# Inverting the softmax sums of three head pairs as 128x9, gathered and spread by transfers

## The reference, cut to what matters

```python
B, H, S, D = 4, 8, 576, 64
scores = q @ k^T / 8 + min(bias(s), 0), causal
attn = exp(scores - max(scores, -1))
attn = attn / (sum(attn, -1) + 1e-9)           # the division that the change is about
x = attn @ v                                    # [B, S, 512]
h = relu(x @ w_in); conv_out = conv over 3 rows of h
x = (h * sigmoid(conv_out)) @ w_out             # 1024 hidden columns
u = x + (x^T @ U @ V)^T
out = u + relu(u @ w_ch1) @ w_ch2               # 2048 hidden columns
```

## Time and profile before

| | us |
|---|---|
| median of 3 runs (998.87 to 1003.27) | 1002.07 |
| the profiled execution | 999.37 |
| its span, first to last instruction | 997.6 |

### The profile page before, as it was taken

How to read it: one execution, slowest core, us unless ns; L and a number is a source line. 1 busy time by engine, 2 the same in 40 slices (tenths; PEclk the granted TensorE clock), 3 DMA queues, 4 the chain that set the end, 5 groups by cost and what they waited for, 6 DMA issues and landing times.

```text
span 997.6 us, 16111 instructions
## 1 busy us (share of the span) xinstructions
PE 929.6 (93%) x6455; PEld 868.0 (87%) x6455; DVE 531.9 (53%) x913; ACT 350.8 (35%) x670; POOL 5.9 (1%) x20
## 2 busy tenths in 40 slices
PE   2898898979999899999999999999999989999998
PEld 1676788968999799987999999987999989889998
DVE  5459896346775583346554784146655670342222
ACT  1365564444333443433332453332332331211111
POOL 1000000000000000000000000000000000000000
PEclk9799997989999799999999999999999999999999
DMA  4677455735564646533645546433555434344441
GB/s 93 137 213 189 110 165 171 214 101 157 179 205 153 180 127 211 191 120 129 186 163 170 169 130 207 154 112 113 177 169 169 170 127 162 127 136 173 167 162 58
DMA packets 68257, 155.68 MB, mean 156 GB/s; under 512 B 30356, under 2 KB 44692, under 8 KB 55896
## 3 DMA queue, kind: packets, MB, share of 16 engines
q1 hardware_dynamic: 68184, 154.66, 49.9%
HBM read 114.57 MB, written 30.03 MB: 145 GB/s over the span
## 4 chain that ended last, share of the span: by engine, by line
PE 75%; DVE 13%; issue 3%; ACT 3%; DMA 2%; SPq 2%; ACTq 0%; DVEq 0%
PE psum L1019 20%; PE psum L1021 18%; PE psum L1020 18%; PE psum L996 8%; PE psum L942 3%; PE psum L975 2%; DVE sums L746 2%; PE psum L973 2%; DVE neg_max L733 2%; DVE work L784 2%; DVE work L787 2%; PE psum L956 1%; DVE work L782 1%; DMA klc<-cum_scratch 1%; DVE ring L844 1%
## 5 line engine op out<-in xcount | busy, mean ns | idle before, releaser
L1019 PE MATMUL psum<-r_hl,ring 128*128 128x288 f32 x512 | 157.7, 308 | 3.8 <-DVE work L816 1.9
L1019 PE MATMUL psum<-uu_hl,ring 128*128 128x288 f32 x512 | 155.8, 304 | 3.1 <-DVE ybuf L806 1.7
L1021 PE MATMUL psum<-r_hl,ring 128*128 128x288 f32 x512 | 152.2, 297 | 0.0
L1020 PE MATMUL psum<-r_hl,ring 128*128 128x288 f32 x512 | 152.2, 297 | 0.0
L1021 PE MATMUL psum<-uu_hl,ring 128*128 128x288 f32 x512 | 151.3, 296 | 0.0
L1020 PE MATMUL psum<-uu_hl,ring 128*128 128x288 f32 x512 | 151.2, 295 | 0.0
L733 DVE TENSOR_REDUCE neg_max<-psum 128x1 f32<-128x512 f32 (+4 forms) x165 | 83.1, 538 | 117.6 <-PE psum L947 110.9
L825 DVE SCALAR_TENSOR_TENSOR r_hl<-psum,r_hl 128x288 fp32r<-128x288 f32 x128 | 58.2, 456 | 154.5 <-ACT r_hl L646 154.3
L996 PE MATMUL psum<-probs,va 128*128 128x320 f32 (+4 forms) x448 | 126.0, 392 | 0.4 <-ACT probs L572 0.4
L646 ACT ACTIVATE r_hl<-psum 128x288 fp32r<-128x288 f32 x128 | 52.4, 411 | 203.8 <-PE psum L1021 203.8
L1019 PEld LDWEIGHTS psum<-r_hl,ring 128*128 128x128 f32 x512 | 97.6, 191 | 7.3 <-DVE work L816 3.1
(11 more groups left out here) (96 smaller groups left out, 1717.4 us busy)
## 6 DMA issues: line engine op xcount, KB each, us to landing
ring<-w_scratch SPq DMA_DIRECT2D x72, 1024.0 KB, 4.9
w_scratch<-ring SPq DMA_DIRECT2D x24, 1024.0 KB, 5.3
kq_raw<-in_kq_t SPq DMA_DIRECT2D x70, 288.0 KB, 4.4
stage<-in_w_ch SPq DMA_DIRECT2D x16, 512.0 KB, 6.7
khc<-khh SPq DMA_DIRECT2D x34, 144.0 KB, 2.3
qm<-qhl SPq DMA_DIRECT2D x34, 144.0 KB, 2.5
out_t<-u_acc SPq DMA_DIRECT2D x16, 288.0 KB, 2.1
va<-in_v SPq DMA_DIRECT2D x34, 128.0 KB, 3.8
```

The costliest lines, as they stand in the source:

```text
L1019: pe.matmul(o, hi, m_hi, start=start, stop=False)
L1020: pe.matmul(o, hi, m_lo, start=False, stop=False)
L1021: return pe.matmul(o, lo, m_hi, start=False, stop=stop)
```

## The change

For pairs 0, 1 and 2 each head's sums now leave PSUM as one row of 576 (one partition instead of 64). SP cuts the rows of the two heads into 64 pieces of 9 and puts them on 128 partitions (`gather_sums`); DVE inverts that 128x9 tile (`invert_few`); SP stores it to DRAM (`store_few`), waits until it is there, and reads each head's row back to all 64 partitions of its half (`spread_few`, two transfers); DVE multiplies the pair's 128x576 at once (`normalise_few`). Pair 3 keeps its two halves with the old code. `sums` has two buffers instead of four, and the split of pair 2 moves from step (7, 1) to (7, 2).

The places: `gather_sums` at step 0 of heads 1 to 6 on SP; `invert_few` in DVE's `then` at step 2 of heads 2, 4 and 6, ahead of `query_low`; `store_few` at step 3 of these heads, behind `load`; `spread_few` at step 4, ahead of `load_v`; `normalise_few` in `then` at step 1 of heads 3, 5 and 7.

```diff
+        few = [sb(f"few{i}", [P, SP9], F32) for i in range(2)]     # SP9 = S // D = 9
+        spread_out = sb("spread_out", [P, S], F32)
-        sums = sb("sums", [P, NPAIR, S], F32)
+        sums = sb("sums", [P, 2, S], F32)
-        X_SPLIT = {(5, 2): 0, (6, 1): 1, (7, 1): 2}
+        FEW_HEADS = (2, 4, 6)
+        X_SPLIT = {(5, 2): 0, (6, 1): 1, (7, 2): 2}
...
+                def gather_sums(a, h):
+                    m, x = a * (NPAIR - 1) + h // 2, h % 2
+                    sp.wait_ge(evict.sem, evict.value(a * H + h))
+                    row = sums[D * (1 - x):D * (1 - x) + 1, h // 2 % 2, :]
+                    sp.dma_start(few[0][x * D:(x + 1) * D, :], row).then_inc(few_in.sem, 16)
+                def store_few(a, pair):
+                    sp.wait_ge(few_done.sem, few_done.value(a * (NPAIR - 1) + pair))
+                    sp.dma_start(few_scratch[a * NPAIR + pair].rearrange("x (p c) -> (x p) c", p=D), few[1][:, :])\
+                      .then_inc(few_out.sem, 16)
+                def spread_few(a, pair):
+                    m = a * (NPAIR - 1) + pair
+                    sp.wait_ge(few_out.sem, few_out.value(m))
+                    norm.wait(sp, a * NPAIR + pair - 1)
+                    for x in range(2):
+                        row = few_scratch[a * NPAIR + pair][x:x + 1, :]
+                        sp.dma_start(spread_out[x * D:(x + 1) * D, :], row.broadcast_to([D, S])).then_inc(spread_in.sem, 16)
                 def attention_step(a, h, g):
+                    if g == 0 and 1 <= h <= 6:
+                        gather_sums(a, h - 1)
                     if g == 2:
                         side(a, h + 2)
                     if g == 3:
                         load(a, h + 3)
+                    if g == 3 and h in FEW_HEADS:
+                        store_few(a, FEW_HEADS.index(h))
+                    if g == 4 and h in FEW_HEADS:
+                        spread_few(a, FEW_HEADS.index(h))
                     if g == 4:
                         load_v(a, h + 2)
...
-                    norm.wait(act, m - NPAIR)
-                    act.activation(sums[o:o + D, h // 2, :], psf[sm:sm + D, O0:O0 + S], ACT.Identity, bias=EPS).then_inc(evict.sem, 1)
+                    norm.wait(act, m - 2)
+                    if h // 2 < NPAIR - 1:
+                        act.activation(sums[sm:sm + 1, h // 2 % 2, :], psf[sm:sm + 1, O0:O0 + S], ACT.Identity, bias=EPS)\
+                           .then_inc(evict.sem, 1)
+                    else:
+                        act.activation(sums[o:o + D, h // 2 % 2, :], psf[sm:sm + D, O0:O0 + S], ACT.Identity, bias=EPS)\
+                           .then_inc(evict.sem, 1)
...
+                def invert_few(a, pair):
+                    m = a * (NPAIR - 1) + pair
+                    dve.wait_ge(few_in.sem, few_in.value(m))
+                    if m:
+                        dve.wait_ge(few_out.sem, few_out.value(m - 1))
+                    dve.reciprocal(few[1][:, :], few[0][:, :]).then_inc(few_done.sem, 1)
+                def normalise_few(a, pair):
+                    x = x_raw[:, pair, :]
+                    evict.wait(dve, a * H + 2 * pair + 1)
+                    dve.wait_ge(spread_in.sem, spread_in.value(a * (NPAIR - 1) + pair))
+                    dve.tensor_tensor(x, x, spread_out[:, :], ALU.mult).then_inc(norm.sem, 1)
...
                 def then(a, h, g):
-                    if g >= 3 and 4 <= h <= 6:
-                        normalise(a, h - 4, g - 3)
+                    if g == 2 and h in FEW_HEADS:
+                        invert_few(a, FEW_HEADS.index(h))
+                    if g == 1 and h - 1 in FEW_HEADS:
+                        normalise_few(a, FEW_HEADS.index(h - 1))
```

More of the change, by code:

```diff
@@ L79, in attention_and_ffn_program @@
     w_scratch = nc.dram_tensor("w_scratch", (BLOCKS, P, 2 * PIECE), F32, kind="Internal").ap()
+    few_scratch = nc.dram_tensor("few_scratch", (B * H // 2, 2, S), F32, kind="Internal").ap()
     cum_scratch = nc.dram_tensor("cum_scratch", (B * H, 2, S), F32, kind="Internal").ap()
@@ L128, in attention_and_ffn_program @@
         max_split = sb("max_split", [P, NT, P], F32R)
-        sums = sb("sums", [P, NPAIR, S], F32)
+        sums = sb("sums", [P, 2, S], F32)
+        SP9 = S // D
+        few = [sb(f"few{i}", [P, SP9], F32) for i in range(2)]
+        spread_out = sb("spread_out", [P, S], F32)
         x_raw = sb("x_raw", [P, NPAIR, S], F32)
@@ L178, in attention_and_ffn_program @@
         evict = Count(sem("evict"), 2, 1)
+        few_in = Count(sem("few_in"), 32)
+        few_done = Count(sem("few_done"), 1)
+        few_out = Count(sem("few_out"), 16)
+        spread_in = Count(sem("spread_in"), 32)
         recip = Count(sem("recip"), 2)
-        norm = Count(sem("norm"), 1, 4)
+        norm = Count(sem("norm"), 1, 2)
         xh_done = Count(sem("xh_done"), 1, 1)
@@ L740, in maxima @@
                                           ALU.subtract).then_inc(ms_lo.sem, 1)
+                def invert_few(a, pair):
[9 more added lines that the diff above has]
+                    dve.tensor_tensor(x, x, spread_out[:, :], ALU.mult).then_inc(norm.sem, 1)
                 def normalise(a, pair, half):
-                    m = a * NPAIR + pair
-                    x, total = x_raw[:, pair, cols(half)], sums[:, pair, cols(half)]
+                    x, total = x_raw[:, pair, cols(half)], sums[:, pair % 2, cols(half)]
                     evict.wait(dve, a * H + 2 * pair + 1)
                     dve.reciprocal(total, total).then_inc(recip.sem, 1)
-                    recip.wait(dve, m, half + 1)
+                    recip.wait(dve, a, half + 1)
                     mul = dve.tensor_tensor(x, x, total, ALU.mult)
```

## The result

| | before | after |
|---|---|---|
| median, us (runs) | 1000.47 (4) | 1012.73 (4) |
| ratio of after to before | | 1.0135, 95% interval 1.010 to 1.017 |
| span of the profiled execution, us | 997.6 | 1010.7 |
| mean granted clock of TensorE | 0.971 | 0.963 |

The change makes the kernel about 1.3% slower. The forecast was 1014 us within 1000 to 1027. The profiled execution of after took 1012.48 us, against the 1011.6 summed for it.

What follows compares the result with a forecast made beforehand. Bound taken: small waits among PE, ACT, DVE and SP in batch 0's attention, PE in later stages. +15.4 + 5 + 0.5 - 4.7 - 4 = +12.2 on 999.4 gives 1011.6; with the median 2.7 higher, 1014 us, range 1000 to 1027.

Steps and rivals of the forecast that it cites:

- The stalls, +15.4: Batch 0, heads 3, 5 and 7: DVE waits for the small transfers, costing 5.4, 5.0 and 5.0 us.
- four stages: Head 3's 5.4 us: gather wait, store landing at 66.0, spreads landing at 69.5, maxima at 70.3 instead of 64.91.
- The clock, +5: Batch 0: PE standing in each stall lowers its granted clock; 5 us for the three together.
- The upper end: Most that the slowed clock could add per stall in batch 0: 5.1 us, from 14.02 against 8.96.
- the lower end of the stalls: Batch 0, pairs 1 and 2: no wait at the gather, so 3.75 us per stall.
- The relief in batch 0, -4.7: Heads 5 to 7 lose what they take beyond 8.96 us as reciprocals and multiplications go: at most 4.7 us.
- The later batches, +0.5 - 4: Batches 1 to 3: 0.5 us lost to SP waiting; 4 us won by lighter DVE in batches 2 and 3.
- SP's hold: SP stands at step 4 until the store lands, up to 4 us; taken as 0.5 us in later batches.
- the rival of a slip in batch 1: Batch 1's weight pipeline slips behind spread_few: up to 10 us on top, 1024 us; chance 0.12.
- The sum: Whole kernel: +15.4 + 5 + 0.5 - 4.7 - 4 = +12.2 us, so 1011.6 for the profiled execution.
- The rival of the draw: Batch 0: small transfers do not queue, each stall costs 2.1 us, the clock holds; 1000 us, chance 0.16.

Runs made afterwards that it cites:

- e4_warm: Changed kernel with 80 more warming matmuls ahead of max_transpose in heads 3, 5 and 7 of batch 0; 1013.87 us, ratio 1.014.
- e1_free: Kernel before with reciprocals of pairs 0 to 2 over only 9 of each half's 288 columns, no transfers added; 995.18 us, ratio 0.9948.
- e5_split: Kernel before with only the split of pair 2 moved from step (7, 1) to (7, 2); 1003.09 us, ratio 1.002.
- e6_from1: Batch 0 as in the kernel before, with four buffers of sums; batches 1 to 3 as in the changed kernel; 994.7 us, ratio 0.998.
- e3_store_first: Changed kernel with the store of inverted sums issued ahead of the load of kq_raw at step 3; 1006.32 us, ratio 1.0068.
- e10_gather_warm: Changed kernel with the gather at step 4, ahead of the weights, and 80 more warming matmuls in heads 3, 5, 7 of batch 0; 1015.55 us, ratio 1.016.
- e12_from1_again: Second measurement of the kernel with batch 0 as before and the change from batch 1 on; 995.39 us, ratio 0.9965.

## Why the prediction was right

**The stalls, +15.4.** Right in mechanism and place, and near in size. Head 3 was worked out in four stages: the wait at the gather 1.65 us (measured 1.68), the store landing 3.9 us after its issue (4.1), the spreads 2.3 us after the last issue (2.7), the last round of maxima 5.4 us later than before (70.48 - 64.91 = 5.6, and 6.2 counting that head 2 came 0.64 us earlier here). Heads 3, 5 and 7 are longer than 8.96 by 6.6, 5.5 and 4.7: 16.8 us. Of the 6.6 some 0.5 is the transposition at half clock, 1.28 us where it is 0.75 in head 7.

**The clock, +5.** Undersized. Heads 4 and 6 are longer than 8.96 by 3.6 and 3.8, and the head behind the third stall is 0.6 longer than in before: some 8 us. The upper end, 5.1 us for a slow head, was read from head 1 of before; that head holds two waits of PE besides the slow clock, of 2.19 and 1.50 us. The reciprocals of pairs 1 and 2 did not wait for their gathers at all, since the slow heads gave these their time; this was named as the lower end of the stalls, and e4_warm shows the exchange.

**The relief in batch 0, -4.7.** Oversized. e1_free wins 2.4 us there, from one execution to the other. Taking everything beyond 8.96 as the reciprocals' doing was the step that failed: of the disturbed heads only head 6 came down, from 12.27 to 8.73, and head 5 kept its 0.9, of which some 0.7 is PE's wait for side transfers. Head 7 went up to 10.6 in that execution, where PE waits 1.80 us for side transfers.

**The later batches, +0.5 - 4.** Near: the ruler gives -4.2, of which e5_split shows 2.3 (head 1 of batch 2) to be that one execution's, and 1.6 more lies in the end, 233.8 us in after and 235.3 or 235.4 in every other run, so that is one execution's too. e6_from1 and its repetition put the true worth at 2 to 3.5 us. That SP's hold costs nothing there is borne out, and the rival of a slip in batch 1 with it: batch 1's eight heads differ by 0.9 us between the two kernels.

**DVE.** 0.208 us for the 128x9 reciprocal (0.15 taken), 0.751 for the multiplication (0.8).

**The sum.** The parts come to +13.1 where +12.2 was forecast, and part of that is luck. Batch 0 was forecast at +15.7 and its heads 3 to 7 measured +19.5 (-0.6 ahead of them): too little was given to clock and stalls. The later batches and the end were forecast at -3.5 and measured -5.8, through gains that are partly one execution's. The two errors cancel.

**The rival of the draw.** It asked for short transfers. The store takes 2.0 us when it stands ahead of `kq_raw` (e3_store_first) and 4.1 in the changed kernel's order. The Trainium skill, "DMA: Bandwidth & Descriptors", section "Anatomy of one DMA", gives about 2.0 us as the fixed part of one DMA, fitted on the path through GpSimd; the trace agrees for the store that stands ahead, 2.0 us, and not for the one behind 576 KB, 4.1.

What stays open: how much of the 19.5 us is stall and how much clock, as shares that could be taken off one at a time. e4_warm shows that they are not additive. Open too is why the same weights land after 6.8 us in one execution and 8.3 in another.

## What to carry to other kernels

A round trip through small transfers costs the queue ahead of each of them, not its bytes: 2.2 KB took 5.8 to 8.0 us behind 1.5 MB, and 4.5 KB took 4.1 us behind 576 KB and 2.0 ahead of it. Before moving work from an engine to transfers, find for each one what is issued just ahead of it and how many microseconds lie between it and its reader, stage by stage; the same change lost some 16 us by the ratios (19.5 from one profiled execution to the other) where a head of five steps took 9 us, and won 2 to 3.5 where it took 20 to 36. And bound the gain first by leaving the work out: here that bound was 5 us, for 44 us off an engine that was busy half the time.

## What the runs showed that was not expected

Removing an idle stretch of PE in order to keep the clock up gave nothing back (e4_warm, 1.014 against 1.0135), because the heads that then ran at full clock met the same transfers earlier. A filler also costs its own length wherever the stall that it was meant for has moved: in e10_gather_warm the maxima were ready before it began, and its 5.18 us, at full clock, went onto head 3, which took 20.2 us. And the order of the transfers does not fix the time of a head: code and issue times alike, head 5 of batch 0 took 9.94 us in before and 13.98 in e12_from1_again, where 512 KB of weights took 1.5 us longer to land. A ruler from one execution must be read with such draws in mind.
